# Three-layer mixer kernel: the low-weight products of the 64 rest rows of two output chunks, each on 64 rows of TensorE's array

## The reference, cut to what matters

```
u  = x + h.transpose(0, 2, 1)                       # second stage, after mixing the tokens
h2 = np.maximum(u @ w_ch1, 0.0) @ w_ch2             # w_ch1 is 320 x 1536, w_ch2 1536 x 320
...
un = (u - mu) / np.sqrt(var + 1e-06)                # third stage, after two Fourier transforms
ch = np.maximum(un @ w_ch1, 0.0) @ w_ch2            # w_ch1 is 320 x 1280, w_ch2 1280 x 320
```

## Time and profile before

| | |
|---|---|
| median of 3 runs | 376.29 us (374.38 to 376.66) |
| profiled execution, own time | 376.1 us |
| its span, first to last instruction | 374.3 us |
| PE busy / PEld busy | 98% / 94% of the span |
| DVE / ACT / POOL busy | 51% / 40% / 29% |
| granted TensorE clock over the span | 1.000 |
| matmuls of `layer1_part` | 88 chunks x 8 = 704, each 128 rows, 384 columns |

### The profile page before, as it was taken

The page is one execution under the profiler, slowest core; times in us unless marked ns, Lnnn a source line. Parts: engine busy times, 40 slices in busy tenths (PEclk is TensorE's granted clock), DMA queues, the critical chain, the costliest instruction groups (busy, mean ns, idle before and its releaser), DMA issues.

```text
span 374.3 us, 6123 instructions
## 1 busy us (share of the span) xinstructions
PE 365.3 (98%) x2371; PEld 353.0 (94%) x2371; DVE 190.4 (51%) x403; ACT 147.9 (40%) x309; POOL 108.4 (29%) x112
## 2 busy tenths in 40 slices
PE   8898999999999999999999999999999999999997
PEld 3788987999999999999999999999999999999996
DVE  7878753653442443134961387537945475431421
ACT  5678788577453132002351134605405302330310
POOL 6248778556333000000025400543514100000000
DMA  7968999543130000004032100605041101001000
GB/s 160 253 179 222 236 313 246 159 121 104 45 106 21 19 1 0 19 2 144 1 107 70 54 0 2 229 32 180 2 148 47 35 3 49 6 0 51 4 19 35
DMA packets 17488, 32.00 MB, mean 86 GB/s; under 512 B 2524, under 2 KB 7780, under 8 KB 17460
## 3 DMA queue, kind: packets, MB, share of 16 engines
q1 hardware_dynamic: 16388, 30.04, 28.3%
q0 software_dynamic: 352, 1.31, 1.3%
q10 hardware_dynamic: 720, 0.27, 0.4%
HBM read 26.99 MB, written 4.62 MB: 84 GB/s over the span
## 4 chain that ended last, share of the span: by engine, by line
PE 83%; ACT 4%; DMA 2%; DVE 1%; issue 1%; SPq 0%; ACTq 0%; DVEq 0%
PE ps L681 31%; PE ps L658 24%; PE ps L661 4%; PE ps L660 4%; PE ps L616 3%; PE ps L540 3%; PE ps L783 3%; PE ps L516 2%; PE ps L764 2%; PE ps L634 2%; DMA og<-in_o 2%; PE ps L525 2%; PE ps L594 1%; PE ps L550 1%; PE ps L502 1%
## 5 line engine op out<-in xcount | busy, mean ns | idle before, releaser
L969 ACT ACTIVATE h_hi<-ps 128x384 fp32r<-128x384 f32 x88 | 43.3, 492 | 121.2 <-PE ps L661 121.2
L1213 DVE SCALAR_TENSOR_TENSOR h_lo<-ps,h_hi 128x384 fp32r<-128x384 f32 x88 | 48.8, 555 | 53.4 <-ACT h_hi L969 52.9
L681 PE MATMUL ps<-ch_hi,h_hi 128*128 128x320 f32 x144 | 45.5, 316 | 0.0
L1219 DVE TENSOR_TENSOR xt<-ps,xt 128x320 f32<-128x320 f32 x24 | 11.8, 490 | 65.3 <-PE ps L681 65.3
L681 PE MATMUL ps<-ch_hi,h_lo 128*128 128x320 f32 x144 | 44.5, 309 | 0.0
L681 PE MATMUL ps<-ch_lo,h_hi 128*128 128x320 f32 x144 | 44.5, 309 | 0.0
L681 PE MATMUL ps<-m_hi,h_hi 128*128 128x320 f32 x120 | 37.4, 312 | 0.0
L681 PE MATMUL ps<-m_hi,h_lo 128*128 128x320 f32 x120 | 37.1, 309 | 0.0
L681 PE MATMUL ps<-m_lo,h_hi 128*128 128x320 f32 x120 | 37.1, 309 | 0.0
L658 PE MATMUL ps<-uT_hi,ch_hi 128*128 128x384 f32 x96 | 33.0, 344 | 0.3 <-DVE xt L1382 0.3
L658 PE MATMUL ps<-uT_lo,ch_hi 128*128 128x384 f32 x96 | 32.1, 335 | 0.0
(11 more groups left out here) (168 smaller groups left out, 861.0 us busy)
## 6 DMA issues: line engine op xcount, KB each, us to landing
kq<-in_kq SPq DMA_DIRECT2D x24, 192.0 KB, 4.6
ch_raw<-in_ch SPq DMA_DIRECT2D x11, 384.0 KB, 6.2
vk<-in_vk SPq DMA_DIRECT2D x12, 328.0 KB, 4.7
m_raw<-in_m SPq DMA_DIRECT2D x11, 320.0 KB, 4.5
og<-in_o SPq DMA_DIRECT2D x12, 160.0 KB, 4.7
x_scratch<-xt SPq DMA_DIRECT2D x12, 160.0 KB, 1.8
out<-xt SPq DMA_DIRECT2D x12, 160.0 KB, 1.8
tok_raw<-in_tok SPq DMA_DIRECT2D x4, 384.0 KB, 6.7
```

The source lines that it names most:

```text
L681: mm = pe.matmul(bank, h[hx][:, f, i * P:(i + 1) * P], w[wx][:, f], start=(f == 0 and hx == 0 and wx == 0), stop=(f == FCH[k] - 1 and hx = ...
L969: act.activation(h[0][:, f], h_bank(k, f), ACT.Relu).then_inc(hhi_done, 1)
L1213: dve.scalar_tensor_tensor(out=h[1][:, f], in0=h_bank(k, f), scalar=0.0, in1=f32(h[0][:, f]), op0=ALU.max, op1=ALU.subtract).then_inc(hlo_ ...
L1219: dve.tensor_tensor(xt[:, tile], o_bank(n), xt[:, tile], ALU.add).then_inc(o_done, 1)
```

## The change

`uT_h` is a new tile of 128 partitions by 384 that has the high parts of the 64 rest channels in both halves. `uT_x` stays as it was, and is still written by two engines: ACT writes its partitions 0 to 63 (a new instruction, counted by a new semaphore `ux_done`) and then `uT_h`; DVE writes its partitions 64 to 127 from `uT_h`.

In `layer1_part` each chunk keeps its six matmuls of full groups and the one with high weights on `uT_x`. The low-weight matmul of 128 rows is gone. In its place, at the end of each chunk with an even number, stand two matmuls of 64 rows each: one on partitions 0 to 63, which adds to the bank of chunk f, and one on partitions 64 to 127, which begins the bank of chunk f + 1. The second waits until that bank is free. Low weights by low input is no longer made for the rest rows.

```diff
+    uT_h = at("uT_h", R_S + 1280, [P, TOK], F32R)
...
                 if f == 0:
                     pe.wait_ge(ulo_done, KC * (k + 1))
+                    pe.wait_ge(ux_done, k + 1)
...
-                i = 0
+                i = f % 2
                 for dc in range(2):
                     for wx, ux in ((0, uT_hi), (0, uT_lo), (1, uT_hi)):
                         pe.matmul(bank, w[wx][:, f, dc * P:(dc + 1) * P], ux[:, dc], start=(i == 0), stop=False)
                         i += 1
-                pe.matmul(bank, w[0][:, f, 2 * P:3 * P], uT_x[:, :], start=False, stop=False)
-                pe.matmul(bank, w[1][:, f, 2 * P:3 * P], uT_x[:, :], start=False, stop=True).then_inc(l1_done, 1)
+                mm = pe.matmul(bank, w[0][:, f, 2 * P:3 * P], uT_x[:, :], start=False, stop=(f % 2 == 1))
+                if f % 2 == 0:
+                    for j in range(2):
+                        half = slice(64 * j, 64 * j + 64)
+                        if j == 1 and k == NBLK:
+                            lo_split(pe, N_DFT + ((f + 2) * KC * P - 1) // 640)
+                        if j == 1 and (k > 0 or f >= 2):
+                            pe.wait_ge(hlo_done, n - 1 if f >= 2 else FBASE[k])
+                        if j == 1 and k == NBLK - 1 and f in (0, 2):
+                            pe.wait_ge(r_done, f + 2)
+                        pair = pe.matmul(h_bank(k, f + j), w[1][half, f + j, 2 * P:3 * P], uT_h[half, :],
+                                         start=(j == 1), stop=(j == 0))
+                        if j == 0:
+                            pair.then_inc(l1_done, 1)
+                else:
+                    mm.then_inc(l1_done, 1)
...
                 for dc in parts:
                     act.wait_ge(tr_done, KC * k + dc + 1)
-                    act.activation(uT_hi[:, dc] if dc < 2 else uT_x[:, :], TR_BANK[k][dc][:, 0:TOK],
+                    if dc == 2:
+                        act.activation(uT_x[0:64, :], TR_BANK[k][dc][0:64, 0:TOK], ACT.Copy).then_inc(ux_done, 1)
+                    act.activation(uT_hi[:, dc] if dc < 2 else uT_h[:, :], TR_BANK[k][dc][:, 0:TOK],
                                    ACT.Copy).then_inc(uhi_done, 1)
...
-                        dve.tensor_tensor(uT_x[64:P, :], src[64:P, 0:TOK], f32(uT_x[64:P, :]),
+                        dve.tensor_tensor(uT_x[64:P, :], src[64:P, 0:TOK], f32(uT_h[64:P, :]),
                                           ALU.subtract).then_inc(ulo_done, 1)
```

More of the change, by code:

```diff
@@ L248, in build @@
     st_x2 = [sem("st_x2_0"), sem("st_x2_1")]
+    ux_done = sem("ux_done")
     gate_step, reset_ready, ea_ready, ah_done, ab_hi = (
```

## The result

The changed kernel takes 387.1 us (median of 4 runs, 386.41 to 388.13) against 375.81 us before (median of 4). The ratio is 1.0306, 95% interval 1.0277 to 1.0335. The forecast was 370.4 us, so both the sign and the range (368.8 to 384.8) missed. The time lies 0.1 us from the upper end of the rival "the array is emptied at each change of shape" (382.5 to 387.2).

What follows compares the result with a forecast made beforehand. PE's back-to-back layer 1 matmuls were taken to bound the kernel: 376.1 us less 6.0 saved by 44 pairs, plus 0.3 lost to other waits, gives 370.4 us; range for 8 in 10, 368.8 to 384.8.

Steps and rivals of the forecast that it cites:

- the array is emptied at each change of shape: Layer 1 pairs: full matmuls and halves wait for each other's end, 0.146 to 0.252 us longer a pair; chance 0.26.
- What bounds the kernel: PE, busy 98% of the span with 83% of the chain; removing a 0.174 us layer 1 matmul slot shortens the run.
- The price of the pair: Layer 1, 44 pairs: two 64-row matmuls take 0.212 us instead of two slots of 0.348, saving 0.136 each.
- I take the second, 6.0 us.: Second of four cases: both loads run from the full matmul's start, second half 0.038 us late; 44 pairs save 6.0 us.
- side by side at once: Layer 1 pairs: second half starts with the first, saving 0.174 us a pair, 7.6 us in all, 369.1 us; chance 0.12.
- the sign of being wrong that the prediction had named: The forecast is wrong if the first full load behind a pair starts late; no size given.
- Its deciding point (0.136 a pair for both waits): Emptied array: it decides against the change once the two waits of a pair come to more than 0.136 us.
- The row on 104 rows: Profile row where PE passes from 128 to 104 rows with no gap; evidence against the emptied array, called weak.
- Fewer rows alone buy nothing: Eight matmuls of 104 rows take 0.86 us, as eight of 128 do; the gain needs halves lying side by side.
- The costs put at nothing: ACT's extra 0.5 us copy at 8 turns and the second half's wait for chunk f + 1's bank: cost 0.
- What falls due instead: Waits on DVE in block 3 and at the end of block 4 take back 0.3 us (0.14 to 0.7).

Runs made afterwards that it cites:

- the run with 96 rows of 384 columns: Kernel before, with the low-weight rest product on partitions 0 to 95 instead of 128 in all 88 chunks: 375.58 us, ratio 0.9993.
- the run with full rows: Changed kernel, same order, waits and extra ACT copy, but both matmuls of a pair on all 128 rows: 375.37 us against 375.33, ratio 1.0011.
- the version that does gain: Kernel before, low-weight rest products of chunks 0 to 7 gathered into one four-pair stretch in blocks 2, 4, 5, 6, 7: 374.03 us against 375.74.

## Why the prediction was wrong, point by point

**What bounds the kernel** was right. PE carries the chain as before, and each 0.1 us in a pair of chunks reached the end: 44 x 0.254 = 11.2 us by block 7 against 11.3 measured.

**The price of the pair** is the step that failed: "I take the second, 6.0 us." It rested on the sentence that it "asks only that a load for free rows need not wait for the matmul before it". The prediction expected the first half at 0.174 us after the full matmul ahead, both loads hidden under it, and the next full load hidden too. The halves do lie side by side, even better than it said (0.00 us apart at the timeline's resolution and not 0.04, the loads too), so that inside a stretch the value of a pair is the full slot of the rival "side by side at once". What fails is the overlap of the loads with the matmul ahead: at a change of shape, in and out, the next load starts 0.27 us after the last matmul's start and not with it, and nothing hides its 0.11 us. The late full load behind a pair is the sign of being wrong that the prediction had named. The term of -44 x 0.136 = -6.0 us is in truth +44 x 0.254 = +11.2 us.

**The rival that came true** had a chance of 0.26 against 0.30 for the forecast. Its mechanism was right and its parts were not. It took the wait as long as the matmul's modelled end, 0.334 us, which is 0.160 more than a slot; measured are 0.27, or 0.10 more. Of the loads it kept the full matmul's hidden, and at its upper end counted 0.106 for the second half's load; in truth that one costs nothing, and the first load on each side is exposed, 0.11 each. Gaps too long by 0.06 on each side and one exposed load too few cancel: 0.252 a pair against 0.254 measured. That the time lies 0.1 us from its upper end is luck. Its deciding point (0.136 a pair for both waits) was passed threefold, 0.40.

**The weighing.** The trace before had no row with 64 rows, so nothing in it could price the step. The row on 104 rows was called weak, rightly: 96 rows pass without a gap too. It is weaker still for "Fewer rows alone buy nothing", since both groups compared there have 84 columns and go at the pace of the loads, 0.106 us; the run with 96 rows of 384 columns shows it at full width, 0.17 us a slot. The rule of the Trainium skill, "TensorEngine Tiling (Array Packing)", Key Properties, that a change of tiling mode drains TensorE, was the only statement that the prediction had on exactly this step. The traces agree as far as they go: at 44 of 44 pairs the first load comes 0.27 us after the start of the matmul ahead, though that is still before its modelled end at 0.34. Where the trace is silent and a stated rule speaks against the change, it should have had more than a quarter. The range, cut in the middle of that rival, shows the same fault. The other rule used, of the Trainium skill, "TensorE: Matmul & The Clock Gate", Part 3, The mechanism, on loads and matmuls of other row groups lying side by side, fits the traces too, within a stretch (0.00 us apart).

**The costs put at nothing** were nothing. ACT's extra copy at 8 turns, the wait in the pair and the moved product together give 1.0011 in the run with full rows. **What falls due instead** hardly came up, since PE was later and not sooner. The stall before chunk 2 of block 3 is 0.22 us in the changed kernel, against 0.27 in the earlier trace rows:

```profile
225.32 0.41 PE L661 MATMUL ps<-uT_hi,ch_hi 128*128 128x384 f32 x1 [0.22 <-DVE xt L1401]
```

It shrank where the prediction had it grow by 0.1 to 0.2; PE came later by its first pair, which fits, but no run separates that. In the version that does gain, block 4 takes 13.64 us (250.93 to 264.57) as block 7 does, and no new wait appears behind it.

## What to carry to other kernels

In this kernel half-array matmuls do run side by side, but the way into such a stretch and out of it costs about 0.2 us each, more than the slot of 0.174 us that one pair saves. Count stretches before counting saved slots: here, by the rule above, a stretch has to hold three pairs to pay (four did), and how many it can hold is set by the PSUM banks that are free. For other types and widths the price was not measured. If a trace has no example of the instruction form that a change introduces, measure one such visit alone before building on it.

## What the runs showed of the hardware that was not expected

- A single 64-row matmul in a stream of full ones costs 0.389 us more than a full one in its place (88 of them: +34.2 us), and a second one on the other 64 rows is then free.
- The wait ends 0.27 us after the last matmul's start, before that matmul's modelled end at 0.334, and it holds back the load, which is then paid in full (0.11 us). Which part of the array or of its queue makes the 0.27 us was not tried.
- 96 rows behave as 128: ratio 0.9993.
